# First-weight products by one level of Strassen with seven products, and the batches in two groups, in an attention and two-layer feed-forward kernel on Trainium2

## The chip, the cores and the metric

The kernel runs on one core of one Trainium2 chip. The metric is device time in microseconds (us). Engines are named as in the profile: PE is TensorE (PEld its weight loads), DVE is VectorE, ACT is ScalarE, POOL is GpSimd, and SP (SPq) issues the DMAs.

## The reference

```python
kv = einsum('bhsd,bhse->bhde', k, v)           # batch 4, heads 8, seq 576, head_dim 64
out = einsum('bhsd,bhde->bhse', q, kv)
out = out / sqrt(mean(out * out, -1) + 1e-6) * g_norm
x = out as (2304 tokens, 512)
h = x @ w_in;  x = (h * sigmoid(h)) @ w_out    # layer 1: 512 -> 2048 -> 512
x = ((x @ w_a) * (x @ w_b)) @ w_out2           # layer 2: 512 -> 1536 (twice) -> 512
```

All tensors are float32. On the chip every feed-forward product is made of three matmuls of type fp32r: each operand is split into a rounded high part and a rest, and high*high, high*rest and rest*high are summed.

## The kernel before

**Attention** comes first, for all 18 token tiles of 128 (PE loop at L460): q is transposed (L344), K^T V is made per head pair (L330), multiplied with q (L358), normalised on DVE and ACT, and transposed back (L369) into xT, which holds the 2304 tokens as 6 blocks of 384. K^T V and q times K^T V are plain float32 matmuls; each appears as two instructions in the trace.

**Weights** are loaded by SP (L230) and split by POOL (L309 rounds to the high part, L311 subtracts for the rest), 68 units of 128x512, each once. Both parts stay in SBUF for all blocks.

**Layer 1** runs block by block. For each of 16 slices of 128 hidden columns, the hidden product (L383) is 12 matmuls of 384 columns into one PSUM bank; ACT takes the sigmoid (L546), DVE multiplies (L680), ACT rounds (L551), DVE subtracts (L683), and 12 matmuls (add1, L408) add the slice's share of the output into four PSUM banks that hold the block's sum. The hidden product runs two slices ahead of add1. **Layer 2** is the same with two hidden products per slice (w_a, w_b), 12 slices, and an output product (L434 to L436) of 9 matmuls of 512 columns per slice in which the tokens are the stationary side. Between blocks ACT rounds the next x (L540) and DVE forms its rest (L674). The results are stored by SP.

In all, the hidden products of layer 1 are 1152 matmuls of 384 columns (16 slices x 6 blocks x 12), those of layer 2 1728, add1 1152, and layer 2's output 648 of 512 columns.

## Time and profile before

| | us |
|---|---|
| median of 3 runs (lowest, highest) | 950.91 (947.35, 951.45) |
| span of the profiled execution | 950.9 |
| first matmul of the output product of layer 1 | 97.99 |
| last matmul starts | 947.37 |

The profiled execution's own time is its span, 950.9 us, and it equals the median. The profile gives for each engine the time in which it was busy, and for groups of like instructions the number, the mean duration and what ended the idle time before them. A matmul's row lasts longer than the distance to the next one's start, because matmuls are pipelined; what a matmul costs in a stream is the distance between starts.

### The profile page before, as it was taken

Reading aid. Unit: us, or ns where it says so; the run is one execution under the profiler, and the core shown is the slowest. Engines: PE = TensorE matmul, PEld = TensorE weight load, DVE = VectorE, ACT = ScalarE, POOL = GpSimd, SP = SyncE. Lnnn points to the kernel's source line nnn. Section 1 sums busy time; section 2 is a strip of 40 time slices with the busy share of each in tenths; the row PEclk is TensorE's granted clock in tenths of the full one; section 3 lists DMA queues with packets and bytes.
Section 4 is the critical chain, followed back from the end, with each engine's and each line's share of the span. In section 5 each row is a group of like instructions: output and inputs, shape, how many; then the busy total and the mean of one; then the engine's idle time right before and its main releaser. Section 6 shows DMA issues by size and latency. Waiting matters only on the chain.

```text
span 950.9 us, 13550 instructions
## 1 busy us (share of the span) xinstructions
PE 922.1 (97%) x5368; PEld 885.4 (93%) x5368; DVE 267.4 (28%) x492; ACT 239.6 (25%) x480; POOL 135.9 (14%) x142
## 2 busy tenths in 40 slices
PE   4988899999999999999999999999999999999998
PEld 3977899999999999999989999999999999999997
DVE  1467323223224223233232122112112112112111
ACT  2354323223223223222222122112112112112111
POOL 0039880000000000007990000000000000000000
PEclk8898999999999999999999999999999999999999
DMA  9984440000000000003430000001000000000000
GB/s 218 257 189 125 120 122 1 0 0 0 0 0 0 0 0 0 0 0 88 123 111 1 1 1 33 0 0 33 0 0 33 0 0 33 0 0 8 26 1 34
DMA packets 41881, 37.06 MB, mean 39 GB/s; under 512 B 4224, under 2 KB 36992, under 8 KB 41856
## 3 DMA queue, kind: packets, MB, share of 16 engines
q1 hardware_dynamic: 41856, 36.71, 14.8%
q8 instruction: 18, 0.29, 0.1%
q14 instruction: 7, 0.06, 0.0%
HBM read 31.98 MB, written 4.72 MB: 39 GB/s over the span
## 4 chain that ended last, share of the span: by engine, by line
PE 91%; SPq 3%; DMA 2%; DVE 2%; issue 1%; ACT 1%; ACTq 0%
PE ps L376 25%; PE ps L378 24%; PE ps L377 24%; PE ps L435 5%; PE ps L436 5%; PE ps L434 5%; SPq L245 1%; SPq L237 1%; DMA q_sb<-in_q_dram 1%; DMA v_sb<-in_v_dram 1%; PE ps L358 1%; PE ps L330 1%; DVE x_lo L674 1%; DVE stat L653 0%; PE ps L344 0%
## 5 line engine op out<-in xcount | busy, mean ns | idle before, releaser
L680 DVE TENSOR_TENSOR gate<-gate,ps 128x384 f32<-128x384 f32 x168 | 93.1, 554 | 383.3 <-ACT gate L546 383.3
L546 ACT ACTIVATE gate<-ps 128x384 f32<-128x384 f32 x168 | 82.7, 492 | 394.9 <-PE ps L378 394.9
L376 PE MATMUL ps<-x_hi,w_hi_top 128*128 128x384 f32 x504 | 169.9, 337 | 1.6 <-DVE x_lo L674 1.6
L378 PE MATMUL ps<-x_hi,w_lo_top 128*128 128x384 f32 x504 | 169.4, 336 | 0.0
L377 PE MATMUL ps<-x_lo,w_hi_top 128*128 128x384 f32 x504 | 169.2, 336 | 0.0
L683 DVE TENSOR_TENSOR g_lo<-gate,g_hi 128x384 fp32r<-128x384 f32 x168 | 94.5, 563 | 245.3 <-ACT g_hi L551 245.3
L376 PE MATMUL ps<-x_hi,w_hi_low 128*128 128x384 f32 x456 | 153.8, 337 | 2.3 <-DVE x_lo L674 2.3
L378 PE MATMUL ps<-x_hi,w_lo_low 128*128 128x384 f32 x456 | 153.1, 336 | 0.0
L377 PE MATMUL ps<-x_lo,w_hi_low 128*128 128x384 f32 x456 | 153.0, 336 | 0.0
L551 ACT CAST g_hi<-gate 128x384 fp32r<-128x384 f32 x168 | 86.3, 514 | 252.0 <-PE ps L378 139.0
L376 PEld LDWEIGHTS ps<-x_hi,w_hi_top 128*128 128x128 f32 x504 | 95.1, 189 | 5.0 <-DVE x_lo L674 2.2
L377 PEld LDWEIGHTS ps<-x_lo,w_hi_top 128*128 128x128 f32 x504 | 95.2, 189 | 1.5
L378 PEld LDWEIGHTS ps<-x_hi,w_lo_top 128*128 128x128 f32 x504 | 95.0, 189 | 0.0
L376 PEld LDWEIGHTS ps<-x_hi,w_hi_low 128*128 128x128 f32 x456 | 86.0, 189 | 4.4 <-POOL w_lo_low L311 1.7
L377 PEld LDWEIGHTS ps<-x_lo,w_hi_low 128*128 128x128 f32 x456 | 86.0, 189 | 1.0
L378 PEld LDWEIGHTS ps<-x_hi,w_lo_low 128*128 128x128 f32 x456 | 86.0, 189 | 0.0
L309 POOL TENSOR_SCALAR w_hi_low<-stage 128x512 fp32r<-128x512 f32 x32 | 20.6, 644 | 355.6 <-PE ps L378 293.5
L376 PE MATMUL ps<-g_hi,w_hi_low 128*128 128x384 f32 x192 | 64.8, 338 | 2.4 <-DVE g_lo L683 2.4
L377 PE MATMUL ps<-g_lo,w_hi_low 128*128 128x384 f32 x192 | 64.9, 338 | 0.0
L378 PE MATMUL ps<-g_hi,w_lo_low 128*128 128x384 f32 x192 | 64.8, 337 | 0.0
L378 PE MATMUL ps<-g_hi,w_lo_top 128*128 128x384 f32 x192 | 64.2, 334 | 0.0
L376 PE MATMUL ps<-g_hi,w_hi_top 128*128 128x384 f32 x192 | 64.1, 334 | 0.0
(59 smaller groups left out, 1071.1 us busy)
## 6 DMA issues: line engine op xcount, KB each, us to landing
stage<-in_moe_w_out_dram SPq DMA_DIRECT2D x28, 256.0 KB, 2.6
k_sb<-in_k_dram SPq DMA_DIRECT2D x16, 288.0 KB, 9.1
v_sb<-in_v_dram SPq DMA_DIRECT2D x16, 288.0 KB, 11.0
stage<-in_moe_w_in_dram SPq DMA_DIRECT2D x16, 256.0 KB, 2.7
q_sb<-in_q_dram SPq DMA_DIRECT2D x4, 768.0 KB, 11.5
stage<-in_moe_w_a_dram SPq DMA_DIRECT2D x12, 256.0 KB, 2.8
stage<-in_moe_w_b_dram SPq DMA_DIRECT2D x12, 256.0 KB, 2.9
out_dram<-xT SPq DMA_DIRECT2D x3, 768.0 KB, 3.3
```

Source lines behind the costliest of these rows:

```text
L237: sp.dma_start(dst[0:KVP, B % 2, 2 * h:2 * h + 2, :], src[B, 2 * h:2 * h + 2].rearrange("h (p t) d -> p h (t d)", t=KVT)).then_inc(kv_in[B ...
L309: nc.gpsimd.tensor_scalar(unit_hi(slot), raw, 1.0, 0.0, ALU.mult, ALU.add).then_inc(w_raw_hi, 1)
L376: pe.matmul(dst, hi[:, cols], moving_hi, start=start, stop=False)
L377: pe.matmul(dst, hi[:, cols], moving_lo, start=False, stop=False)
L378: return pe.matmul(dst, lo[:, cols], moving_hi, start=False, stop=stop)
L434: pe.matmul(dst, g_hi[:, f % 2, cols], unit_hi(slot), start=(f == 0), stop=False)
L435: pe.matmul(dst, g_hi[:, f % 2, cols], unit_lo(slot), start=False, stop=False)
L436: mm = pe.matmul(dst, g_lo[:, f % 2, cols], unit_hi(slot), start=False, stop=(f == F2 - 1))
L546: nc.scalar.activation(gate[:, f % 2, :], ps[:, bank, 0:TOK], func).then_inc(s_ready, 1)
L551: nc.scalar.copy(g_hi[:, f % 2, :], gate[:, f % 2, :]).then_inc(gh_ready, 1)
L680: nc.vector.tensor_tensor(gate[:, f % 2, :], gate[:, f % 2, :], ps[:, bank, 0:TOK], ALU.mult).then_inc(g_full, 1)
L683: nc.vector.tensor_tensor(g_lo[:, f % 2, :], gate[:, f % 2, :], g_hi[:, f % 2, :].bitcast(F32), ALU.subtract).then_inc(g_ready, 1)
```

## The change

The feed-forward part is written anew, and the attention with it.

- **Two groups.** Batches 0 and 1 (1152 tokens) go through attention, layer 1 and layer 2, then batches 2 and 3. The attention of the second group stands inside the pairs 1 to 5 of layer 2 of the first group (PE lines L547 to L580). Every weight is loaded and split twice, once for each group.
- **Strassen.** A hidden product covers a pair of hidden slices (256 columns), the 512 inputs in two halves, and a group's tokens in two halves of 576 (its batches). One level of Strassen (Winograd's form) turns the eight block products into seven. Each of the seven steps (`step`, L419) is 12 matmuls of 288 columns. POOL makes the sums of weights (L324, L327, L330, L337) and splits each of the seven operands (L311, L313) into a ring of four; DVE makes the four sums of x and the seven rests once per layer and group (L833, L837), ACT rounds them (L656). ACT keeps partial sums from PSUM (L683, 3 per product) and DVE adds them (L870, 3 per product).
- **Output products** have no PSUM sum over slices any more: after each pair a tile (6 matmuls, of 288 columns at L467 to L469 in layer 1, of 512 at L489 to L491 in layer 2) goes to one of two banks, and DVE adds it to the running sum in SBUF (L919, L929). Layer 1 has 16 tiles per pair, layer 2 nine.
- Layer 1 has 8 pairs per group, layer 2 has 6 pairs with two products each. The matmuls of all hidden products are 1344 of 288 columns in layer 1 and 2016 in layer 2; the output products are 1536 of 288 and 648 of 512.

The core of the diff:

```diff
-            def hidden(bank, slot, x_first):
-                for c in range(KT):
-                    if x_first is not None:
-                        pe.wait_ge(x_ready, x_first + c + 1)
-                    mm = three(ps[:, bank, 0:TOK], weights(slot), slice(c * P, (c + 1) * P),
-                               x_hi[:, c, :], x_lo[:, c, :], c == 0, c == KT - 1)
-                return mm
...
+    SEGS = [(g, layer) for g in range(GROUPS) for layer in (1, 2)]
+    N_PAIRS = [FF1 // (2 * P) if layer == 1 else FF2 // (2 * P) for _, layer in SEGS]
...
+    STEPS = 7
+    RING = 4
+    RAWS = 2
+    G_HALVES = 3
+    BANK_A, BANK_B, BANK_C, BANK_D = 0, 2, 4, 6
+    STEP_BANK = (BANK_A, BANK_A, BANK_A, BANK_B, BANK_A, BANK_C, BANK_C)
+    STEP_BEGINS = (0, 3, 5)
...
+                n = max(n for n in range(len(SEGS)) if RAW0[n] <= r)
+                layer = SEGS[n][1]
+                p, what = divmod(r - RAW0[n], layer + 1)
+                if what == layer:
+                    sp.wait_ge(d_ready, 2 * (PAIR0[n] + p + 1))
+                else:
+                    sp.wait_ge(w_sum, 4 * (PROD0[n] + layer * p + what + 1))
...
+            def load_heads(G, h):
+                buf, fill = staged(G, h)
+                if G and h == 0:
+                    sp.wait_ge(x_ready, 2 * STEPS)
+                before = PAIRS * G + h - (2 if G == 0 else 1)
+                if before >= 0 and (G, h) != (1, 0):
...
+            for r in range(2, RAW0[-1]):
+                load_raw(r)
+                h, rest = divmod(r - RAW0[1], 3)
+                if rest == 2 and 0 <= h < PAIRS:
+                    load_heads(1, h)
+                if r == RAW0[2] + 5:
+                    sp.wait_ge(flushed, DOWN0[2])
+                    for j in range(TOK_TILES):
+                        store_tile(0, j)
...
+            def ready(u, step, src):
+                n = STEPS * u + step
+                if n >= RING:
+                    pool.wait_ge(prod, n - RING + 1)
+                nc.gpsimd.tensor_scalar(w_hi[:, n % RING], src, 1.0, 0.0, ALU.mult, ALU.add).then_inc(w_high, 1)
+                pool.wait_ge(w_high, n + 1)
+                nc.gpsimd.tensor_tensor(w_lo[:, n % RING], src, w_hi[:, n % RING].bitcast(F32),
+                                        ALU.subtract).then_inc(w_ready, 1)
+            def up(u):
+                r = raw_up(u)
+                pool.wait_ge(raw_in[r % RAWS], 16 * (r // RAWS + 1))
+                w = raw[:, r % RAWS, :].rearrange("p (c n) -> p c n", c=KT)
+                b11, b12, b21, b22 = (w[:, 2 * i:2 * i + 2, j * P:(j + 1) * P] for i in range(2) for j in range(2))
+                t0, t1, t2 = (wt[:, j, :].rearrange("p (c n) -> p c n", c=2) for j in range(3))
+                if u:
+                    pool.wait_ge(w_ready, STEPS * u)
+                nc.gpsimd.tensor_tensor(t0, b12, b11, ALU.subtract).then_inc(w_sum, 1)
+                ready(u, 0, b11)
+                pool.wait_ge(w_sum, 4 * u + 1)
+                nc.gpsimd.tensor_tensor(t1, b22, t0, ALU.subtract).then_inc(w_sum, 1)
+                pool.wait_ge(w_sum, 4 * u + 2)
+                ready(u, 1, t1)
+                nc.gpsimd.tensor_tensor(t2, b22, b12, ALU.subtract).then_inc(w_sum, 1)
+                ready(u, 2, t0)
+                ready(u, 3, b21)
+                ready(u, 4, b22)
+                pool.wait_ge(w_sum, 4 * u + 3)
+                ready(u, 5, t2)
+                pool.wait_ge(w_ready, STEPS * u + 3)
+                nc.gpsimd.tensor_tensor(t0, b21, t1, ALU.subtract).then_inc(w_sum, 1)
+                pool.wait_ge(w_sum, 4 * u + 4)
+                ready(u, 6, t0)
...
+                if pp >= 2:
+                    pool.wait_ge(down, down_end(pp - 2))
...
+                at = (STEPS * u + n) % RING
+                pe.wait_ge(w_ready, STEPS * u + n + 1)
+                if u == PROD0[seg]:
+                    pe.wait_ge(x_ready, STEPS * seg + n + 1)
+                if n in STEP_BEGINS and u:
+                    if layer == 2 and u == prods_of(pp)[1]:
+                        if n == 0:
+                            pe.wait_ge(a_kept, a_count(pp))
+                        else:
+                            pe.wait_ge(added, 3 * (u - 1) + (1 if n == 3 else 3))
+                    else:
+                        pe.wait_ge(g_ready, 4 * (pp - 1) + {0: 2, 3: 1, 5: 4}[n])
+                if n in (1, 2):
+                    pe.wait_ge(part_kept, 3 * u + n)
+                if n == 4:
+                    pe.wait_ge(part_kept, 3 * u + 3)
+                if n == 6:
+                    pe.wait_ge(added, 3 * u + 2)
+                bank, begins = STEP_BANK[n], n in STEP_BEGINS
+                for c in range(2):
+                    hi, lo = w_hi[:, at, c, :], w_lo[:, at, c, :]
+                    for w, x, first, last in ((hi, x_hi, c == 0, False), (hi, x_lo, False, False),
+                                              (lo, x_hi, False, c == 1)):
+                        for s in range(2):
+                            mm = pe.matmul(ps[:, bank + s, 0:PART], w, x[:, n, c, s * PART:(s + 1) * PART],
+                                           start=(begins and first), stop=last, skip_group_check=not begins)
+                mm.then_inc(prod, 1)
...
+                t = down0(pp) + n
+                m, d, s = down_order(pp)[n]
+                bank, at = tile_bank(t), (2 * pp + m) % G_HALVES
...
+                wait_turn(bank)
+                part, cols = slice(at * SEQ + s * PART, at * SEQ + (s + 1) * PART), slice(d * P, (d + 1) * P)
...
+                for n in range(STEPS):
+                    step(u, n)
+                    down1(before, 2 * n)
+                    down1(before, 2 * n + 1)
+                down1(before, 14)
+                down1(before, 15)
...
+                step(ua, 0)
+                tile(0)
+                step(ua, 1)
+                tile(1)
+                step(ua, 2)
+                if old is not None:
+                    o_turn(1, old, 0, 6)
+                    o_turn(1, old, 1, 7)
+                step(ua, 3)
+                if new is not None:
+                    kv(1, new)
+                step(ua, 4)
+                tile(2)
+                if old is not None:
+                    o_turn(1, old, 2, other(2))
+                step(ua, 5)
+                tile(3)
+                step(ua, 6)
+                if new is not None:
+                    q_turn(1, new, 0, 6)
+                    q_turn(1, new, 1, 7)
+                step(ub, 0)
+                tile(4)
+                step(ub, 1)
+                tile(5)
+                step(ub, 2)
+                if new is not None:
+                    q_turn(1, new, 2, 6)
+                    q_kv(1, new, 0, 7)
+                step(ub, 3)
+                if new is not None:
+                    q_kv(1, new, 1, 6)
+                step(ub, 4)
+                tile(6)
+                step(ub, 5)
+                tile(7)
+                step(ub, 6)
+                if new is not None:
+                    q_kv(1, new, 2, other(8))
+                tile(8)
...
+                    act.wait_ge(flushed, DOWN0[seg] - 4)
+                x_round(seg, 0, quad(G, 0, 0))
+                act.wait_ge(x_sum, 4 * seg + 2)
+                x_round(seg, 1, ts[1])
+                x_round(seg, 2, ts[0])
...
+                act.wait_ge(prod, STEPS * u + n + 1)
+                if u:
+                    act.wait_ge(added, 3 * (u - 1) + (1, 3, 2)[n])
+                nc.scalar.copy(halves(kept[:, n, :]), both(BANK_A)).then_inc(part_kept, 1)
...
+                x_add(ts[0], quad(G, 1, 0), quad(G, 1, 1), ALU.add)
+            def x_second(seg):
+                G = SEGS[seg][0]
+                ts = [mat(kvq0, j) for j in range(3)]
+                dve.wait_ge(x_sum, 4 * seg + 1)
+                x_add(ts[1], ts[0], quad(G, 0, 0), ALU.subtract)
+                x_rest(seg, 0, quad(G, 0, 0))
+            def x_third(seg):
+                G = SEGS[seg][0]
+                ts = [mat(kvq0, j) for j in range(3)]
+                x_rest(seg, 1, ts[1])
+                x_rest(seg, 2, ts[0])
+                x_add(ts[2], quad(G, 0, 1), ts[1], ALU.subtract)
+                x_rest(seg, 3, quad(G, 0, 1))
+                x_rest(seg, 4, ts[2])
+                x_add(ts[0], quad(G, 0, 0), quad(G, 1, 0), ALU.subtract)
+                x_rest(seg, 5, ts[0])
+                x_rest(seg, 6, quad(G, 1, 1))
...
+                bank, at, n = ((BANK_B, 0, 3), (BANK_C, 2, 5), (BANK_C, 1, 6))[which]
+                dve.wait_ge(prod, STEPS * u + n + 1)
+                dve.wait_ge(part_kept, 3 * u + at + 1)
+                nc.vector.tensor_tensor(dst, halves(kept[:, at, :]), both(bank), ALU.add).then_inc(added, 1)
...
+            def g_rest(pp, tile):
+                m, f = ((0, 0), (0, 1), (1, 1), (1, 0))[tile]
+                dve.wait_ge(g_high, 4 * pp + tile + 1)
...
+                nc.vector.tensor_tensor(halves(g_at_half(g_lo, pp, m, f)), place(tile),
+                                        halves(g_at_half(g_hi, pp, m, f)).bitcast(F32),
+                                        ALU.subtract).then_inc(g_ready, 1)
...
+                def flush(n):
+                    if plain:
+                        flush1(before, n)
+                for n in range(6):
+                    flush(n)
+                add(u, 0, both(BANK_B))
+                flush(6)
+                silu(pp, 0)
+                flush(7)
+                g_rest(pp, 0)
+                silu(pp, 1)
+                flush(8)
+                flush(9)
+                g_rest(pp, 1)
+                add(u, 1, halves(held[:, 2, :]))
+                flush(10)
+                flush(11)
+                silu(pp, 2)
+                g_rest(pp, 2)
+                flush(12)
+                add(u, 2, both(BANK_C))
+                flush(13)
+                flush(14)
+                silu(pp, 3)
+                flush(15)
+                g_rest(pp, 3)
...
+                if layer == 1:
+                    for n in range(8):
+                        flush1(last, n)
+                    dve.wait_ge(flushed, DOWN0[seg + 1] - 8)
+                    x_first(seg + 1)
+                    for n in range(8, 12):
+                        flush1(last, n)
+                    dve.wait_ge(flushed, DOWN0[seg + 1] - 4)
+                    x_second(seg + 1)
+                    for n in range(12, 16):
+                        flush1(last, n)
+                    dve.wait_ge(flushed, DOWN0[seg + 1])
+                    x_third(seg + 1)
...
+                    dve.wait_ge(x_kept, 2 * UNITS)
+                    x_first(nxt)
+                    flush2(last, 0)
+                    x_second(nxt)
+                    flush2(last, 1)
+                    x_rest(nxt, 1, ts[1])
+                    flush2(last, 2)
+                    x_rest(nxt, 2, ts[0])
+                    flush2(last, 3)
+                    x_add(ts[2], quad(H, 0, 1), ts[1], ALU.subtract)
+                    x_rest(nxt, 3, quad(H, 0, 1))
```

What the order of the instructions shows. **TensorE at the start of layer 1, before** (ident and normed belong to the attention; g is a slice of the hidden layer):

```order
L378 MATMUL ps<-x_hi,w_lo_low 128x384
L369 MATMUL ps<-ident,normed 128x128 x8
L480 UNCONDITIONAL_BRANCH
L402 ISA
L405 ISA
L376 MATMUL ps<-g_hi,w_hi_low 128x384
```

**TensorE in the second pair of layer 1, with the change** (the end of a step, then two output tiles):

```order
L448 MATMUL ps<-x_hi,w_hi 128x288 x2
L448 MATMUL ps<-x_lo,w_hi 128x288 x2
L448 MATMUL ps<-x_hi,w_lo 128x288 x2
L467 MATMUL ps<-g_hi,d_hi 128x288
L468 MATMUL ps<-g_lo,d_hi 128x288
L469 MATMUL ps<-g_hi,d_lo 128x288
```

Where a matmul of 384 columns stood for each pair of weight and token block, there are now two of 288 for the same weights, and the tiles of the pair before stand between the steps.

**VectorE at the end of a block, before** (ISA and REGISTER_ALU rows are addresses and waits):

```order
L680 TENSOR_TENSOR gate<-gate,ps 128x384
L683 TENSOR_TENSOR g_lo<-gate,g_hi 128x384
L673 ISA
L674 ISA
L674 TENSOR_TENSOR x_lo<-xT,x_hi 128x384
L673 REGISTER_ALU
```

**VectorE from layer 1 to layer 2 of a group, with the change** (kvq_65 now holds the sums of x):

```order
L919 TENSOR_TENSOR xy<-xy,ps 128x288 x8
L833 TENSOR_TENSOR kvq_65<-xy 128x1152
L919 TENSOR_TENSOR xy<-xy,ps 128x288 x4
L833 TENSOR_TENSOR kvq_65<-kvq_65,xy 128x1152
L837 TENSOR_TENSOR x_lo<-xy,x_hi 128x1152
L919 TENSOR_TENSOR xy<-xy,ps 128x288 x4
L837 TENSOR_TENSOR x_lo<-kvq_65,x_hi 128x1152 x2
L833 TENSOR_TENSOR kvq_65<-xy,kvq_65 128x1152
L837 TENSOR_TENSOR x_lo<-xy,x_hi 128x1152
```

Four operations of 384 elements have become eleven of 1152, and the sixteen adds of output tiles stand between them.

**VectorE in the first pair of layer 1, with the change**:

```order
L837 TENSOR_TENSOR x_lo<-xy,x_hi 128x1152
L870 TENSOR_TENSOR ps<-kept,ps 128x2x288
L879 TENSOR_TENSOR ps<-held,ps 128x2x288
L905 TENSOR_TENSOR g_lo<-ps,g_hi 128x576
L879 TENSOR_TENSOR ps<-held,ps 128x2x288
L905 TENSOR_TENSOR g_lo<-ps,g_hi 128x576
L870 TENSOR_TENSOR held<-kept,ps 128x576
```

The second add at L870, for which the seventh step on TensorE waits, stands behind five operations of the first half.

## Rows read from the trace of the kernel before

**Rows 1.** The page: span, and busy time of each engine

```profile
span 950.9 us, 13550 instructions
PE 922.1 (97%) x5368; PEld 885.4 (93%) x5368; DVE 267.4 (28%) x492; ACT 239.6 (25%) x480; POOL 135.9 (14%) x142
PE ps L376 25%; PE ps L378 24%; PE ps L377 24%; PE ps L435 5%; PE ps L436 5%; PE ps L434 5%; SPq L245 1%; SPq L237 1%; DMA q_sb<-in_q_dram 1%; DMA v_sb<-in_v_dram 1%; PE ps L358 1%; PE ps L330 1%; DVE x_lo L674 1%; DVE stat L653 0%; PE ps L344 0%
L376 PEld LDWEIGHTS ps<-x_hi,w_hi_top 128*128 128x128 f32 x504 | 95.1, 189 | 5.0 <-DVE x_lo L674 2.2
```

**Rows 2.** Windows: stretch, its us, busy (instructions) per engine, granted clock, DMA

```profile
112.00:480.00 368.00, 368.00 (x2124) 367.94 (x2123) 113.47 (x207) 101.62 (x207) 71.31 (x73) 1.00 0.09 26
490.00:494.00 4.00, 2.55 (x12) 1.62 (x10) 4.00 (x4) 1.18 (x3) 3.92 (x4) 1.00 0.49 131
494.00:498.00 4.00, 3.83 (x13) 3.77 (x14) 0.99 (x2) 0.00 (x0) 3.83 (x4) 0.57 0.25 66
```

**Rows 3.** Timeline of PE in layer 2: start us, us, instruction

```profile
897.57 0.39 PE L434 MATMUL ps<-w_hi_low,g_hi 128*128 128x512 f32 x1
...
899.65 0.33 PE L376 MATMUL ps<-x_hi,w_hi_low 128*128 128x384 f32 x1
```

**Rows 4.** The same at the end of the kernel

```profile
941.44 0.39 PE L434 MATMUL ps<-w_hi_top,g_hi 128*128 128x512 f32 x1
...
947.37 0.39 PE L436 MATMUL ps<-w_hi_top,g_lo 128*128 128x512 f32 x1
```

**Rows 5.** Timeline of PE in the attention

```profile
24.09 2.43 PE L330 MATMUL ps<-v_sb,k_sb 96*64 96x64 f32 x24 [4.60 <-DMA v_sb<-in_v_dram]
...
35.35 1.43 PE L330 MATMUL ps<-v_sb,k_sb 96*64 96x64 f32 x24
36.71 1.16 PE L358 MATMUL ps<-kv_sb,qT_sb 128*128 128x128 f32 x8
37.70 0.60 PE L369 MATMUL ps<-ident,normed 128*128 128x128 f32 x4
38.14 0.60 PE L344 MATMUL ps<-ident,q_tile 128*128 128x128 f32 x4
38.67 1.09 PE L358 MATMUL ps<-kv_sb,qT_sb 128*64 128x128 f32 x16
```

**Rows 6.** The page's DMA issues, KB each and us to landing

```profile
k_sb<-in_k_dram SPq DMA_DIRECT2D x16, 288.0 KB, 9.1
```

**Rows 7.** Groups by form, DVE and ACT: busy us, mean ns of one, idle before

```profile
L680 DVE TENSOR_TENSOR gate<-gate,ps 128x384 f32<-128x384 f32 x168 | 93.1, 554 | 383.3 <-ACT gate L546 383.3
L700 DVE COPY xT<-ps 128x512 f32 x5 | 3.4, 683 | 0.0
L546 ACT ACTIVATE gate<-ps 128x384 f32<-128x384 f32 x168 | 82.7, 492 | 394.9 <-PE ps L378 394.9
L573 ACT COPY xT<-ps 128x512 f32 x5 | 2.9, 587 | 0.3
```

**Rows 8.** POOL's two lines: duration ns min/median/max, first and last start

```profile
L309 POOL TENSOR_SCALAR w_hi_top<-stage x36: 612/622/928, 97.6 to 501.4; 128x512 fp32r<-128x512 f32 x36
L311 POOL TENSOR_TENSOR w_lo_top<-stage,w_hi_top x36: 1274/1294/1694, 98.3 to 502.1; 128x512 fp32r<-128x512 f32 x36
```

**Rows 9.** DVE's line L674 (ns min/median/max), then its timeline between the layers

```profile
L674 DVE TENSOR_TENSOR x_lo<-xT,x_hi x48: 544/553/1644, 78.9 to 871.1; 128x384 fp32r<-128x384 f32 x48
490.03 4.96 DVE L674 TENSOR_TENSOR x_lo<-xT,x_hi 128x384 fp32r<-128x384 f32 x4
```

**Rows 10.** Timeline of PE, the first matmul of add1

```profile
97.99 0.49 PE L376 MATMUL ps<-g_hi,w_hi_low 128*128 128x384 f32 x1 [2.39 <-DVE g_lo L683]
```

1153 lines of the change are left out of this document (649 added, 504 removed).

## The prediction

> **What bounds the kernel now.** I read the page first. TensorE is busy 97% of the span, VectorE 28%, ScalarE 25%, GpSimd 14%, and the chain that ended last is made of TensorE's feed-forward lines [rows 1]. The windows say how dense the middle is: 2124 matmuls in 368 us, 0.1733 us from start to start at 384 columns, at a granted clock of 1.00 [rows 2]. The timeline gives the other shape: nine matmuls of 512 columns take 2.08 us, 0.231 each [rows 3], at the very end 26 take 5.93 us, 0.228 each [rows 4]. The feed-forward part is then 4032 x 0.1733 + 648 x 0.231 = 848 us. Ahead of it lie 98.0 us [rows 10], in which the attention and the first 36 matmuls (6 us) run, and 3.5 us follow the start of the last matmul. 98.0 - 6 + 848 + 3.5 = 944; the other 7 us are waits and stretches at half clock, such as the one between the layers. So only two things can help: fewer columns, and a shorter stretch before the stream starts. All times below are made against the profiled execution, 950.9 us, which equals the median of the runs. A measurement of this kernel can tell about 0.5% from no change, 4.75 us.
>
> **Term 1, the stream.** The change leaves 1344 + 2016 + 1536 = 4896 matmuls of 288 columns and the 648 of 512. In columns, 1,880,000 become 1,742,000. What a 288-column matmul costs is nowhere in the trace. At 384 columns the distance is 13.3 ns over 384/2.4 = 160, at 512 it is 18 over 213.3 in the middle and 15 at the end [rows 2 to 4]. Either the surplus is a share (0.1733/384 = 0.451 ns a column, which gives 0.2311 at 512, just what the middle shows), or it is a fixed 13 to 15 ns per matmul. The first gives 130.0 ns at 288, the second 133.3. I take 130.0, because the 512-column row of the same stretch bears it out. Ends: 128 (the end's 0.228/512 a column) and 135 (120 + 15).
> 84 of the 4896 belong to the first pair of the first group and are counted in term 2, so the stream is 4812 x 0.130 + 648 x 0.231 = 625.6 + 149.7 = 775 us.
>
> The Trainium skill ("TensorE: Matmul & The Clock Gate", Back-to-back issue gap) gives a warm gap of N/2.4 + 2.5 ns, which would be 122.5 ns at 288. The trace disagrees: at 384 the page's formula gives 162.5 and the row 173.3. With the page's gap the sum would be 36 us lower; the row at 384 leaves that under 1%, counted in A.
>
> **Term 2, up to the second pair.** The first keys land about 9.1 us after their issue [rows 6], so K^T V starts near 10. It is 72 instructions of 64 columns, 0.10 us each at half clock and 0.057 at full [rows 5]; those of the change alternate between the two column halves, and where that happens in the trace (128*64, 16 instructions in 1.09 us) the same columns take half the time of 128*128 (8 in 1.16). First head pair: 4 us for it, 4 more to the end of q times K^T V, 18 in all. Each of the next three head pairs is one chain through all engines, since one sq buffer and one turn of the banks link them: three squares with their sums 3, three copies of q 1.6, last transpose and its copy 0.9, two more copies and three normalisations on VectorE 3.6, transpose back 0.4, q times K^T V 2.5; 12 us, 36 for three. The last one's normalisation and copies 6. x is complete at 60 us.
> VectorE then has three operations of 1152 elements before the first step and eight after it. One costs 0.554 at 384 and 0.683 at 512 [rows 7], 1.0 ns an element, so 1.3 at 1152: 4 + 10. The first pair's seventh step waits for the second add, which stands behind add, two multiplies and two rests of the first half, with ScalarE's sigmoid and rounding between: 6.5; then the step, 1.6. With 2 for GpSimd (below): 60 + 24 = **84 us**. Bounds 74 (a chain of 10) and 98 (15, all at half clock).
>
> **Term 3, the second group's attention in layer 2.** 288 K^T V instructions x 0.0285 = 8.2, 72 transposes x 0.11 = 7.9, 144 of q times K^T V x 0.068 = 9.8 [rows 5]: **26 us** on TensorE, beside which nothing is saved. Upper bound 34 without the overlap.
>
> **Term 4, the steady pairs.** Layer 1: TensorE 84 + 96 matmuls, 23.4 us. VectorE 11 operations of 576 at 0.75 and 16 adds of 288 at 0.45, 15.5. ScalarE 11 at 0.64 (0.492 at 384, 0.587 at 512 [rows 7]), 7. GpSimd, with 256 elements at half of the row plus start-up, 0.36 and 0.68 [rows 8]: 11 x 0.68 + 7 x 0.36 + gaps 1 = 11 per product, and 4 for the output weights, 15. Layer 2: TensorE 34.3, VectorE 16.7, GpSimd 26, ScalarE 7. Work on the three engines is hidden by sum; the order costs something. Written out from the end of the fourth step, VectorE reaches the flush of tile 12 at 11.1 us, when tile 14 wants its bank, and that of tile 13 at 12.2, when tile 15 wanted it at 11.9: 0.3 to 0.65 a pair, 14 pairs, **7 us**. In layer 2 the same exercise gives no wait in plain pairs; in the four with attention tile 6 waits 1.2 for ScalarE's second copy of o, and the weights behind the heads' six DMAs in SP's queue may come late: **8 us**.
>
> **Term 5, the hand-offs.** From layer 1 to 2 of a group TensorE has 16 tiles and 14 steps, 34 us. VectorE needs 16 flushes, 11 operations on x at 1.3, then the adds, and tiles 10 and 14 wait for banks behind it (3 us), steps 2, 3 and 7 of the first product and step 7 of the second wait 8. Beside that stands GpSimd: four operations of 384 took 4.96 us instead of 2.2 while it worked [rows 9], 0.7 each, and all of the eleven have two SBUF operands; where GpSimd's operations are shorter I take 3. **14 us**, twice. From group 1 to group 2 x is split between the last flushes: 7.5 and 3 less overlap, **10 us**. After 2.5 busy of 4 us, TensorE ran 4 us at 0.57 [rows 2], 1.7 lost; three such, **5 us**.
>
> **Term 6, the end**: as before, **3.5 us**.
>
> Sum: 84 + 775 + 26 + 7 + 8 + 28 + 10 + 5 + 3.5 = **947 us**, 0.4% below. The narrower and fewer products save 63 us (4032 x 0.1733 = 699 against 4896 x 0.130 = 636), and the half attention ahead of the stream 19 (92 against 84 less the first pair's 11). The second group's attention, the hand-offs and the order pay back 84, where before had waits of 7.
>
> **Rivals.**
> *A, cheap hand-offs.* TensorE's queue of tiles may cover more than I count: VectorE's back-to-back rows overlap, its share in the steady state is under 70%, the attention chain may keep the full clock. Term 2 then is 76, terms 4 and 5 half: 947 - 8 - 26 = 913 to 935, say **925**. Against it speak the operations' lengths, which are rows.
> *B, a fixed surplus per matmul* (slower). TensorE pays 13.3 ns for each matmul whatever its columns. 4812 x 3.3 ns = 16 us more: **963**. The place is every matmul of 288; it decides from about 132 ns on. For it: the last rows show 15 ns at 512, hardly more than at 384 [rows 4]. Against: the middle shows 18 [rows 3].
> *C, VectorE's order sets layer 1.* If an add into SBUF with one operand in PSUM, or a write to PSUM, costs a fifth more than my rows, each pair waits 1.5 to 2 us, and hand-offs take 18: 947 + 18 + 10 = **975**.
> *D, GpSimd bounds layer 2.* If 256 elements cost nearly what 512 do (0.62 and 1.29), a pair takes 11 x 2 x 1.29 + 14 x 0.62 + 4 = 41 us against TensorE's 34: 12 pairs x 7, **1030**. It decides from about 1.0 us for the subtract. Against: nothing in rows 8 separates start-up from length, but 0.62 is half of 1.29 for the same elements.
> *E, weight loads bound TensorE.* A load's row is 189 ns against a distance of 173 [rows 1]. If loads set the pace, 4812 x 0.173 gives **1150**. Transposes follow at 0.11 us, each with its own load [rows 5], so a load needs no more than that. The Trainium skill ("Perfetto Trace Analysis", Identifying the Most-Contended Engine) says to judge TensorE by MFU and the busy share of LDWEIGHTS; that share is 93% here, and the change adds a fifth to the number of loads, so the rule speaks for this rival and against the change.
>
> **How the numbers follow.** Forecast (938 to 956) 38%, A 24%, B 20%, C 12%, D 4%, E 2%. Of the forecast's own 38, 17 lie below 946.2, 20 within 0.5% and 1 above; A is faster; of B one is within 0.5%; C, D and E are slower. Faster 41 to 42%, same 21%, slower 37%. The cases of both signs hold the chance, so the likeliest one's own range is 938 to 956; the range for 8 in 10 runs from the middle of A, 920, to past C, 982.
>
> **What would show it.** Distance of 288-column starts: 0.130 (B: 0.133). Second pair of layer 1 starting near 84. A steady pair of layer 1 in 24 us, of layer 2 in 34 to 35, about 43 with attention. Between the layers of a group 48 us from the first of the last pair's 16 tiles to layer 2's second pair, with VectorE busy through most of it. GpSimd's 256-element subtract 0.68. The prediction is wrong if pairs are spaced by an engine other than TensorE, if TensorE stays cold in the attention, or if the hand-offs take under 6 us.

## The result, and the profile after

The changed kernel takes 994.58 us (median of 4, 992.8 to 998.61) against 949.25 for the kernel before in the same series (4 runs, 947.35 to 951.45): a ratio of 1.0489, 95% interval 1.0456 to 1.0523. It is slower by 45 us where 947 was forecast, and the time lies 13 us above the upper end of the range. The profiled execution spans 990.7 us at a mean granted clock of 0.96 (before 0.986); the rows below are of it.

The page answers [rows 1]: TensorE's share falls from 97% to 90%. VectorE is busy twice as long as before (549.2 us, before 267.4), GpSimd four times (554.6, before 135.9) and ScalarE a fifth longer (285.7, before 239.6); none of them comes near the span.

```profile
span 990.7 us, 16939 instructions
PE 889.8 (90%) x6552; PEld 835.2 (84%) x6552; DVE 549.2 (55%) x889; ACT 285.7 (29%) x469; POOL 554.6 (56%) x839
PE   4838999999948999999995799999996799999998
L448 PE MATMUL ps<-x_hi,w_hi 128*128 128x288 f32 x1120 | 248.9, 305 | 61.0 <-ACT kept L683 41.9
```

The row of busy tenths shows where TensorE is not full: at the start, and at three places further on, each of which is the beginning of a layer. The last row names what ended most of the idle time: ScalarE's copy of a partial sum (`kept`, L683). The list of waits has the same, with how often and the longest (us in total, times, longest):

```profile
PE ps L448 <- ACT kept L683: 41.9, 13, 10.3
PE ps L448 <- DVE held L870: 14.0, 6, 5.7
PE ps L467 <- DVE xy L919: 5.4, 4, 2.0
PE ps L489 <- DVE xy L929: 4.1, 4, 1.5
PE ps L448 <- POOL w_lo L313: 0.2, 1, 0.2
```

GpSimd, the rival bound of layer 2, costs TensorE 0.2 us. The windows answer [rows 2] (stretch, its us, busy us and instructions per engine, granted clock, DMA): seven pairs of layer 1 from the second on, then the hand-off from layer 1 to layer 2, then the one between the groups.

```profile
88.40:260.00 171.60, 171.45 (x1257) 168.60 (x1256) 104.38 (x190) 50.64 (x78) 104.94 (x157) 0.99 0.15 44
260.00:305.10 45.10, 28.65 (x177) 27.10 (x178) 25.70 (x33) 11.09 (x13) 9.97 (x16) 0.85 0.17 43
530.00:568.20 38.20, 23.99 (x126) 21.12 (x125) 23.30 (x26) 13.58 (x16) 14.10 (x20) 0.83 0.09 28
```

The stream is dense (171.45 of 171.6 us), the hand-offs are not (28.65 of 45.1 us, and the granted clock falls to 0.85). The time went to the hand-offs. A part of it is the clock: by the distances between starts, matmuls at half clock cost TensorE some 15 us more than at full clock from 60 us on, 9.5 of them in the three hand-offs; in the kernel before it was some 5 us.

The timeline of TensorE at the start of the stream shows one of them. The first step runs at half clock (0.24 us a matmul, from 60.16 on); then:

```profile
62.70 0.68 PE L448 MATMUL ps<-x_hi,w_lo 128*128 128x288 f32 x2
71.31 0.82 PE L448 MATMUL ps<-x_hi,w_hi 128*128 128x288 f32 x2 [7.93 <-ACT kept L683]
...
81.52 0.42 PE L448 MATMUL ps<-x_hi,w_lo 128*128 128x288 f32 x2
85.43 0.82 PE L448 MATMUL ps<-x_hi,w_hi 128*128 128x288 f32 x2 [3.49 <-DVE held L870]
```

The second step waits 7.93 us for a copy of 0.63 us. ScalarE's own timeline says why: the copy is behind seven roundings of x (L656), and these wait for VectorE's sums of x.

```profile
63.89 1.15 ACT L656 CAST x_hi<-kvq 128x1152 fp32r<-128x1152 f32 x1 [1.85 <-DVE kvq L833]
68.42 1.15 ACT L656 CAST x_hi<-kvq 128x1152 fp32r<-128x1152 f32 x1 [3.38 <-DVE kvq L833]
69.48 1.15 ACT L656 CAST x_hi<-xy 128x1152 fp32r<-128x1152 f32 x1
70.53 0.63 ACT L683 COPY kept<-ps 128x576 f32<-128x576 f32 x1
```

The program says the same: `x_rounds(seg)` issues all seven roundings before the first `part` of the layer's first product, so the copy that frees the bank for step two cannot leave before the last rounding. Every layer of both groups begins so; the four waits for that copy are 7.93, 10.33, 6.74 and 9.71 us, 34.7 together.

What a matmul costs stands in the timeline of the steady part, where rows 3 gave it for the kernel before:

```profile
91.49 0.29 PE L468 MATMUL ps<-g_lo,d_hi 128*128 128x288 f32 x1
...
92.81 0.30 PE L469 MATMUL ps<-g_hi,d_lo 128*128 128x288 f32 x1
92.94 0.42 PE L448 MATMUL ps<-x_hi,w_hi 128*128 128x288 f32 x2
```

Eleven distances in 1.45 us are 0.132 each. Inside the steps of steady pairs the distances are not all alike: most are 131 to 132 ns, and every fourth is 140, so that the mean is 0.1333. A whole steady pair (180 matmuls) is 24.0 us of 0.1333 and takes 24.43. What makes every fourth one longer no run here tells. Rows 2 had 0.1733 at 384 without such a pattern.

### The profile page after: what moved, and what is told of

Read it like the earlier page. It is cut to its first block, busy times and chain, and to the rows that moved or that the text cites. A ratio compares the mean times of both kernels' runs of the same rounds, so it can differ in the third digit from the quotient of the medians.

```text
span 990.7 us, 16939 instructions
## 1 busy us (share of the span) xinstructions
PE 889.8 (90%) x6552; PEld 835.2 (84%) x6552; DVE 549.2 (55%) x889; ACT 285.7 (29%) x469; POOL 554.6 (56%) x839
## 4 chain that ended last, share of the span: by engine, by line
PE 82%; DVE 10%; ACT 3%; issue 2%; DMA 1%; SPq 1%; POOL 0%; ACTq 0%; DVEq 0%; POOLq 0%
PE ps L448 44%; PE ps L467 8%; PE ps L468 7%; PE ps L469 7%; PE ps L489 5%; PE ps L491 4%; PE ps L490 4%; DVE x_lo L837 3%; DVE kvq L833 2%; PE ps L405 2%; ACT g_hi L707 1%; ACT kept L683 1%; DMA raw<-in_moe_w_a_dram 1%; PE ps L415 1%; PE ps L380 1%
## 5 line engine op out<-in xcount | busy, mean ns | idle before, releaser
L448 PE MATMUL ps<-x_hi,w_hi 128*128 128x288 f32 x1120 | 248.9, 305 | 61.0 <-ACT kept L683 41.9
L448 PEld LDWEIGHTS ps<-x_hi,w_hi 128*128 128x128 f32 x1120 | 187.6, 193 | 76.5 <-issue 66.2
L448 PE MATMUL ps<-x_lo,w_hi 128*128 128x288 f32 x1120 | 245.3, 301 | 0.0
L448 PE MATMUL ps<-x_hi,w_lo 128*128 128x288 f32 x1120 | 243.9, 300 | 0.0
L448 PEld LDWEIGHTS ps<-x_hi,w_lo 128*128 128x128 f32 x1120 | 185.7, 194 | 0.0
L448 PEld LDWEIGHTS ps<-x_lo,w_hi 128*128 128x128 f32 x1120 | 184.8, 194 | 0.0
L311 POOL TENSOR_SCALAR w_hi<-raw 128x256 fp32r<-128x256 f32 x120 | 51.6, 430 | 200.1 <-PE ps L448 200.0
L467 PE MATMUL ps<-g_hi,d_hi 128*128 128x288 f32 x512 | 155.4, 303 | 9.0 <-DVE xy L919 5.4
L683 ACT COPY kept<-ps 128x576 f32<-128x576 f32 x120 | 77.0, 641 | 278.7 <-PE ps L448 278.6
L311 POOL TENSOR_SCALAR w_hi<-wt 128x256 fp32r<-128x256 f32 x160 | 70.5, 441 | 147.3 <-PE ps L448 143.3
L469 PE MATMUL ps<-g_hi,d_lo 128*128 128x288 f32 x512 | 151.3, 295 | 0.0
L468 PE MATMUL ps<-g_lo,d_hi 128*128 128x288 f32 x512 | 151.2, 295 | 0.0
L919 DVE TENSOR_TENSOR xy<-xy,ps 128x288 f32<-128x288 f32 x224 | 99.9, 452 | 89.3 <-PE ps L469 88.6
L313 POOL TENSOR_TENSOR w_lo<-wt,w_hi 128x256 fp32r<-128x256 f32 x160 | 118.5, 741 | 13.4
L467 PEld LDWEIGHTS ps<-g_hi,d_hi 128*128 128x128 f32 x512 | 96.9, 189 | 16.4 <-issue 12.2
L929 DVE TENSOR_TENSOR xy<-xy,ps 128x512 f32<-128x512 f32 x90 | 61.6, 685 | 87.3 <-PE ps L491 87.3
L313 POOL TENSOR_TENSOR w_lo<-raw,w_hi 128x256 fp32r<-128x256 f32 x120 | 98.1, 818 | 10.0
L469 PEld LDWEIGHTS ps<-g_hi,d_lo 128*128 128x128 f32 x512 | 96.5, 189 | 0.0
L489 PE MATMUL ps<-d_hi,g_hi 128*128 128x512 f32 x216 | 86.0, 398 | 5.5 <-DVE xy L929 4.1
L491 PE MATMUL ps<-d_hi,g_lo 128*128 128x512 f32 x216 | 84.6, 392 | 0.0
```

What stands on the lines that cost most here:

```text
L311: nc.gpsimd.tensor_scalar(w_hi[:, n % RING], src, 1.0, 0.0, ALU.mult, ALU.add).then_inc(w_high, 1)
L313: nc.gpsimd.tensor_tensor(w_lo[:, n % RING], src, w_hi[:, n % RING].bitcast(F32), ALU.subtract).then_inc(w_ready, 1)
L448: mm = pe.matmul(ps[:, bank + s, 0:PART], w, x[:, n, c, s * PART:(s + 1) * PART], start=(begins and first), stop=last, skip_group_check=no ...
L467: pe.matmul(dst, hi, g_hi[:, f, part], start=(f == 0), stop=False)
L468: pe.matmul(dst, hi, g_lo[:, f, part], start=False, stop=False)
L469: mm = pe.matmul(dst, lo, g_hi[:, f, part], start=False, stop=(f == 1))
```

## Experiments

Times are medians; each ratio is to the kernel before, run on the same chip in the same series. Theory 1: the overshoot is mostly ScalarE's order at the four layer starts, and 16 us the price of a matmul. Rivals: VectorE's order or the length of its operations on x, the second group's attention, an eighth that Strassen does not save.

**e1_act_order: ScalarE copies the partial sums between the roundings.**

```diff
                 x_round(seg, 2, ts[0])
+                part(PROD0[seg], 0)
...
                 x_round(seg, 3, quad(G, 0, 1))
+                part(PROD0[seg], 1)
...
                 x_round(seg, 4, ts[2])
+                part(PROD0[seg], 2)
```

(and the three copies are left out where the layer's first pair had them)

> ScalarE's three copies of partial sums of a segment's first product now stand between its roundings of x instead of behind all seven. Theory 1 (ScalarE's program order holds the second step back: waits of 7.9, 10.3, 6.7 and 9.7 us on the line of the copies): these four waits shrink to under 2 us each; about 6.5 us at the start, 8.5 between the layers of each group and 5.5 between the groups come off, 29 us in all: about 965 us. Rival 2 (VectorE's eleven operations on x set the hand-off whatever ScalarE does): the waits move to the rests of x and to VectorE's adds, and less than 10 us come off: about 988. Rival 3 (GpSimd's operations delay VectorE's): no change, 994.

Measured: 968.81 us (967.63 to 971.32), ratio 1.0226 [1.0184, 1.0269]: 26 us less than the change. The waits for the copy are down to 0.82 us, of which the copy itself is 0.64:

```profile
64.65 0.82 PE L448 MATMUL ps<-x_hi,w_hi 128*128 128x288 f32 x2 [0.82 <-ACT kept L686]
...
68.69 0.82 PE L448 MATMUL ps<-x_hi,w_hi 128*128 128x288 f32 x2 [0.82 <-ACT kept L686]
```

and its list of waits has another row on top:

```profile
PE ps L448 <- DVE held L875: 18.0, 6, 6.7
PE ps L448 <- ACT kept L686: 9.0, 12, 0.8
```

The copies cost 9.0 instead of 41.9 us; the second add of the first product (`held`) costs 18.0 instead of 14.0. Of the 32.9 us, 26 reach the end. Theory 1 holds for its larger part. What is left over the matmuls in the hand-offs is 19.8 and 17.5 us from layer 1 to layer 2 and some 15 between the groups, where the forecast had 14, 14 and 10.

**e2_dve_add: VectorE makes the second add of a layer's first pair ahead of the first half's multiplies and rests.**

```diff
                 add(u, 0, both(BANK_B))
+                if not plain:
+                    add(u, 1, halves(held[:, 2, :]))
...
-                add(u, 1, halves(held[:, 2, :]))
+                if plain:
+                    add(u, 1, halves(held[:, 2, :]))
```

> In each segment's first pair VectorE makes the second add, for which the seventh step waits, before the multiplies and rests of the first half; ScalarE's order is as in the change. Theory: the waits for this add in the first pair (3.5 and 5.7 us in layer 1, 1.5 twice in layer 2, 12 in all) go, and 1 to 3 us come back in the tiles that wait for the later rests: about 985 us. Rival (these waits lie beside others that are longer): no change, 994.

Measured: 1000.32 us (1000.2 to 1000.49), ratio 1.0563 [1.0521, 1.0606]; 6 us slower than the change, where 985 or no change was expected. A miss. The wait for the add shrinks from 3.49 to 0.94 us, but the next pair now begins with another:

```profile
84.13 0.51 PE L448 MATMUL ps<-x_hi,w_hi 128*128 128x288 f32 x2 [0.94 <-DVE held L870]
...
88.40 0.51 PE L448 MATMUL ps<-x_hi,w_hi 128*128 128x288 f32 x2 [2.45 <-DVE g_lo L905]
```

The rests of the first half (`g_lo`), which the move delayed, are what the next product's first step waits for. In layer 2 the second pair waits 2.24 and 2.53 us for a copy of ScalarE, where it waited 0.59 and 0.84, and gets 1.7 and 3.2 us longer. In this order the chain from the first add to the last rest has no room; what is moved ahead in it delays what stands behind.

**e3_both: the two together.**

```diff
+                part(PROD0[seg], 0)
...
+                if not plain:
+                    add(u, 1, halves(held[:, 2, :]))
```

> Both edits. If the two waits lie one behind the other, their gains add: 994 - 29 - 10 = 955 us. If the second is only another name of the first, the time is that of the first edit alone, about 965. If VectorE's sum of work sets the hand-off, it stays above 980.

Measured: 974.17 us (973.83 to 979.52), ratio 1.0304 [1.0252, 1.0355], 5 us slower than e1_act_order alone and neither of the two values expected (955, 965). In layer 1 the first two pairs together gain 1.9 us in one group and 1.8 in the other; in layer 2 the second pairs lose 3.2 each (45.2 and 39.0 instead of 42.0 and 35.8). It bears e2_dve_add out.

**e5_no_attn2: the second group's attention and its loads left out.**

```diff
-                new = p - 1 if G == 0 and 1 <= p <= PAIRS else None
-                old = p - 2 if G == 0 and 2 <= p <= PAIRS + 1 else None
+                new = None
+                old = None
...
+            nc.vector.memset(xy[:, 1, :], 0.5).then_inc(cleared, 1)
```

> Leaves out the attention of batches 2 and 3 and its loads; their x is a constant. Theory (the second group's attention costs TensorE its own time and little more): pairs 2 to 5 of layer 2 of the first group fall from 41.3 to 42.3 us to 34.7, and the time by 4 x 7.1 + 1, to about 965 us. Rival (it also delays weights or VectorE at the hand-off between the groups): more than 35 us come off, below 959. Rival (it fills gaps and costs little): under 15 us come off.

Measured: 967.3 us (966.89 to 967.72), ratio 1.0215 [1.0161, 1.0268]; 27 us less than the change. Layer 2's pairs with attention take 34.7 to 35.5 us instead of 41.3 to 42.1. The change's own timeline has what a head pair's matmuls take by themselves, here for K^T V, for three transposes, and for a third of q times K^T V:

```profile
331.38 1.28 PE L380 MATMUL ps<-kvq 64*64 64x64 f32 x72
348.38 0.49 PE L393 MATMUL ps<-ident,kvq 128*128 128x128 f32 x3
348.80 0.88 PE L405 MATMUL ps<-kv_sb,qT_sb 128*64 128x128 f32 x12
```

From start to start K^T V takes 1.21 us, the nine transposes of q 0.99, q times K^T V 2.42 and the nine transposes of o 0.82: 5.4 us a head pair, 22 for the four. The other 5 us of the 27 are on top. They are waits (0 to 1.5 us a pair, some of them for ScalarE's copies of o) and larger distances of the matmuls beside the attention (23.1 to 23.4 us for a pair's steps instead of 22.3). In sum the attention costs less than the 26 and 8 us forecast; it is not where the forecast failed.

**e6_flush13: e1_act_order, and in the steady pairs of layer 1 VectorE takes tile 13 from its bank ahead of the third add.**

```diff
                 flush(12)
-                add(u, 2, both(BANK_C))
                 flush(13)
+                add(u, 2, both(BANK_C))
```

> The first edit (ScalarE's copies between the roundings), and in the steady pairs of layer 1 VectorE's flush of tile 13 ahead of the third add. Theory (the 0.43 us by which a steady pair of layer 1 exceeds its 180 matmuls is tile 15 waiting for that flush): 14 pairs fall from 24.43 to 24.0 us, 6 us in all, 963 us. Rival (the 0.43 is made of TensorE's own turns of banks or semaphores): still 24.4, 969.

Measured: 965.88 us (964.81 to 967.36), ratio 1.0198 [1.0173, 1.0222]. It is 3 us less than e1_act_order, where 6 were expected. A steady pair takes 24.14 to 24.20 instead of 24.43 us: the wait that the prediction counted for tile 15's bank (0.3 to 0.65 us a pair) is real, and the order undoes somewhat more than half of it.

**e8_short_rests: e1_act_order, with only 16 of 1152 elements of each rest of x for layer 2.**

```diff
+                if seg in (1, 3):
+                    nc.vector.tensor_tensor(x_lo[:, n, :, 0:8], src[:, :, 0:8], x_hi[:, n, :, 0:8].bitcast(F32),
+                                            ALU.subtract).then_inc(x_ready, 1)
+                    return
```

> The first edit, and VectorE's rests of x for layer 2 (seven of 1152 elements for each group) only 16 elements long; the others keep layer 1's values, so the precision of layer 2 is not that of the reference. Theory (after ScalarE's order is mended, VectorE's work on x holds steps 5 to 7 back): the waits for x and the add behind it (2.6, 1.0 us) go and the clock stays up; each hand-off from layer 1 to 2, 79 us for two pairs, falls to about 71: 969 - 16 = 953 us. Rival (what is left are the copies of partial sums between steps without tiles): less than 6 us come off.

Measured: 957.06 us (956.55 to 957.57), ratio 1.0105 [1.0077, 1.0134]; 12 us less than e1_act_order, where 16 were expected. The two pairs across each hand-off to layer 2 take 70.9 us instead of 79.0 and 76.7, where their matmuls need 59.2. So with ScalarE's order mended, 6 to 8 us of each such hand-off hang on the length of VectorE's seven subtracts, and some 12 are there without them. Matmuls at half clock are a part of the 6 to 8: they cost 4.1 and 1.5 us in these places in e1_act_order's trace, and none run at half clock there in this one.

**e7_early_x: e6_flush13 with work on x moved forward.** The first group's x is rounded and summed in part during its attention, the second group's three sums and two rests are made inside the last pair of layer 2, and the first pairs are ordered add, rest, both multiplies, second add, rests of g. It is a rewrite of some 80 lines; the core:

```diff
+                if last:
+                    dve.wait_ge(x_kept, 2 * UNITS)
+                    x_first(2)
+                    dve.wait_ge(x_sum, 9)
+                    x_add(ts[1], ts[0], quad(1, 0, 0), ALU.subtract)
+                    dve.wait_ge(x_sum, 10)
+                    x_add(ts[2], quad(1, 0, 1), ts[1], ALU.subtract)
...
+                if h == 3:
+                    dve.wait_ge(x_kept, 2 * JS)
+                    x_add(held[:, 0:2, :], quad(0, 0, 0), quad(0, 1, 0), ALU.subtract)
```

> Both edits of the run before, and work on x moved to where VectorE is idle: for the first group one sum and one rounding and rest during the attention; for the second group three sums and two rests during the last pair of layer 2 of the first; in the first pair of layer 1 of each group the adds, multiplies and rests stand between and behind the rests of x, with the second add early and ScalarE's two sigmoids first; tile 8 between the last two steps. Theory (the hand-offs are long because single-engine orders put late what TensorE wants next, not because VectorE's sum of work is too large): the first pair ends near 75 us instead of 87, the hand-off between the groups falls by 12 us, and the time is 963 - 12 - 12 = 939 us, below that of the kernel before. Rival (VectorE with GpSimd beside it is simply too slow there): it stays above 955.

Measured: 951.87 us (7 runs, 949.91 to 956.23), ratio 1.0054 [1.0026, 1.0082]; 14 us less than e6_flush13, 13 short of what was expected and also below the rival's 955. The hand-off between the groups, last pair and first pair, goes from 74.1 to 60.9 us (from 79.9 in the change). The run changes many things at once and does not tell what each of them is worth. The start of the stream gains little:

```profile
63.24 0.82 PE L453 MATMUL ps<-x_hi,w_hi 128*128 128x288 f32 x2 [2.32 <-DVE x_lo L885]
...
77.66 0.50 PE L453 MATMUL ps<-x_hi,w_hi 128*128 128x288 f32 x2 [1.35 <-DVE held L918]
...
85.08 0.49 PE L453 MATMUL ps<-x_hi,w_hi 128*128 128x288 f32 x2 [2.40 <-ACT kept L712]
```

The first pair is 4 us shorter than e6_flush13's, the second 3.4 longer, 28.3 us: its copy (L712) stands behind the last rounding of g in ScalarE's queue. The same mistake one pair on.

**e10_attn_order: e7_early_x with another order in the first group's attention.**

```diff
                 if h + 1 < PAIRS:
                     kv(0, h + 1)
+                if h:
+                    for j in range(JS):
+                        o_turn(0, h - 1, j, j)
...
-                if i:
-                    act.wait_ge(ssq, i)
-                nc.scalar.activation(sq[:], ps[:, bank, 0:TILE3], ACT.Square).then_inc(sq_ready, 1)
+                if i > 2:
+                    act.wait_ge(ssq, i if G else i - 2)
+                nc.scalar.activation(sq_buf(G, j), ps[:, bank, 0:TILE3], ACT.Square).then_inc(sq_ready, 1)
```

> The kernel of e7_early_x with another order in the first group's attention: TensorE transposes a head pair's normalised o back (L420) after the next head pair's q times K^T V instead of before it, ScalarE makes the three squares one after the other into three buffers and copies o after them, and takes the transposed-back tiles of the pair before. Theory: a head pair there is a chain through four engines, about 10 us long, of which 2.5 to 3 us is q times K^T V standing behind the normalisation of the pair before; then three periods get 2 to 3 us shorter each, the first step of the stream starts 6 to 8 us earlier, near 50 us instead of 57.7, and the run takes about 945 us. Rival: the chain is set by the sum of VectorE's work (about 6.3 us a head pair) and waits around it, or by the loads of q, k and v; then nothing or under 3 us comes of it, 949 to 952 us. Against the kernel before neither can be told from no change with certainty: 945 would be 0.2 per cent faster.

Measured: 951.98 us (12 runs, 950.47 to 954.97), ratio 1.0042 [1.0025, 1.0059]: nothing gained, the rival's case. One reason is on the timeline:

```profile
22.04 2.19 PE L413 MATMUL ps<-kv_sb,qT_sb 128*64 128x128 f32 x36
27.36 0.89 PE L388 MATMUL ps<-kvq 64*64 64x64 f32 x40 [3.14 <-DMA kvq<-in_v_dram]
```

TensorE is ready for the third head pair's K^T V some 3 us before v is there; later the copies wait for one another on ScalarE. Which of loads and copies would decide with the other gone was not tried.

**e4_step_twice: the change with each product's fourth step done twice,** as an eighth block product would be.

```diff
-                for c in range(2):
+                for c in (0, 1, 0, 1) if n == 3 else (0, 1):
```

> The change with the fourth step of every product done twice (the second time from a cleared bank, so that the result is the same): eight steps where Strassen has seven. Theory (a step in the stream costs its 12 matmuls, 12 x 0.1333 = 1.6 us, 40 products): 994 + 64 = 1058 us, less what falls into waits of the four first pairs, up to 8: 1050 to 1058. Rival (the three idle engines' work bounds the pairs): under 1030.

Measured: 1060.22 us (1059.61 to 1060.84), ratio 1.1194 [1.1163, 1.1226]; 66 us more than the change. 480 matmuls of 0.1333 us are 64.0, and a steady pair of layer 1 takes 26.03 instead of 24.43 us, 12 matmuls of 0.1333 more. So 0.1333 us is what a matmul of 288 columns costs in this stream. The seventh-for-eighth of Strassen is worth in full what it should be in this kernel; what it saves is spent elsewhere.

**e9_narrow and e11_cols256: e1_act_order with fewer columns in the eight matmuls of a step that hold a rest.**

```diff
+                        cols = PART if w is hi and x is x_hi else 192
                         for s in range(2):
-                            mm = pe.matmul(ps[:, bank + s, 0:PART], w, x[:, n, c, s * PART:(s + 1) * PART],
+                            mm = pe.matmul(ps[:, bank + s, 0:cols], w, x[:, n, c, s * PART:s * PART + cols],
```

> The kernel of e1_act_order in which the eight matmuls of a step that hold a rest (high times rest, rest times high) read and write only 192 of the 288 columns of each half; the other 96 get the product of the high parts alone, so a part of the small terms is left out. 2240 matmuls change. Two theories of a matmul's price. Fixed surplus of 13.3 ns per matmul (rival B of the prediction): the distance from a start to the next is 192/2.4 + 13.3 = 93.3 ns at 192 columns, a step takes 4 x 0.1333 + 8 x 0.0933 = 1.28 us instead of 1.60, a steady pair of layer 1 takes 2.2 us less (about 22.2), and the run is 2240 x 0.040 = 90 us shorter where TensorE sets the pace, about 880 to 890 us if the hand-offs keep their length. A surplus that is a share of the columns (0.451 ns a column from the 384-column row of before, 0.463 from the 288-column row of the change): 87 to 89 ns, steps of 1.23 us, 95 to 105 us shorter. If weight loads set a floor (PEld rows of some 190 ns), distances do not fall under 133 ns at all and the time stays near 969 us.

Measured: 936.04 us (935.73 to 936.35), ratio 0.9867 [0.9832, 0.9902], 33 us less than e1_act_order where 80 to 105 were expected. Both theories miss. The timeline, two matmuls to a row:

```profile
112.23 0.42 PE L449 MATMUL ps<-x_hi,w_hi 128*128 128x288 f32 x2
112.49 0.36 PE L449 MATMUL ps<-x_lo,w_hi 128*128 128x192 f32 x2
112.69 0.39 PE L449 MATMUL ps<-x_hi,w_lo 128*128 128x192 f32 x2
112.91 0.45 PE L449 MATMUL ps<-x_hi,w_hi 128*128 128x288 f32 x2
```

The rows of 192 columns take 0.20 and 0.22 us for two. But the row of 288 columns behind them takes 0.29 instead of 0.26, so the two rows by themselves flatter the price. Over a pair, 56 narrowed matmuls save 1.1 us in layer 1 (23.3 instead of 24.43) and 112 save 2.34 in layer 2 (32.36 instead of 34.70), which leaves 0.112 to 0.113 a matmul, not 0.093. Something else than columns holds them at about the 0.11 us of the transposes [rows 5]. It is not a floor of 0.133, the third case of the expectation. The same edit with 256 in the place of 192 lies above it:

> As e9_narrow, with 256 instead of 192 of 288 columns in the eight matmuls of a step that hold a rest; the other 32 columns of each half get the product of the high parts alone. In e9_narrow the distances at 192 columns came out at 110 to 113 ns, where a fixed surplus gives 93.3 and a share 87 to 89: something of about 111 ns holds each matmul, as in the transposes, which also follow at 0.11 us. 256 columns lie above that by either theory. Fixed surplus: 256/2.4 + 13.3 = 120.0 ns; a share: 0.451 to 0.463 ns a column, 115.5 to 118.5 ns; with the floor added to rather than compared with the columns (a rounding off between the two) 122 to 125 ns. A steady pair of layer 1 has 56 such matmuls: 24.43 - 56 x 0.0133 = 23.7 us by the fixed one, 23.4 to 23.6 by a share; the run about 968.8 - 2240 x 0.0133 = 939 to 950 us.

Measured: 943.73 us (7 runs, 942.15 to 946.27), ratio 0.993 [0.9909, 0.9951], 25 us less than e1_act_order; a steady pair takes 23.65 us.

```profile
112.62 0.42 PE L449 MATMUL ps<-x_hi,w_hi 128*128 128x288 f32 x2
112.88 0.40 PE L449 MATMUL ps<-x_lo,w_hi 128*128 128x256 f32 x2
113.12 0.40 PE L449 MATMUL ps<-x_hi,w_lo 128*128 128x256 f32 x2
113.35 0.43 PE L449 MATMUL ps<-x_hi,w_hi 128*128 128x288 f32 x2
```

Over layer 1's steady stretch the 256-column starts are 118.4 ns apart and the 288-column starts of the same steps 131.8: 13.4 ns for 32 columns, 0.42 a column. The expectation had 120.0 ns for a fixed surplus and 115.5 to 118.5 for a share of the columns, and for the pair 23.7 us and 23.4 to 23.6. The 118.4 ns lie at the upper end of the share's range, the 23.65 us between the two, so the run does not decide. What the distance has over columns/2.4 is 11.7 ns at 256 columns, 11.8 at 288 in this run, 13.3 at 384 and 15 to 18 at 512: neither the same everywhere nor a constant share. In this run the longer fourth distance is missing; in the change it is 140 ns and makes the mean 133.3. The 33 us at 192 columns and 25 at 256 also say that below 256 little more is to be had: 64 columns fewer give 8 us for 2240 matmuls.

No version that computes all that the reference asks for beats the kernel before; the nearest are e7_early_x and e10_attn_order, 0.5% and 0.4% above it. e9_narrow and e11_cols256 are shorter than the kernel before only because they leave small terms out.

## Why the prediction was wrong

The forecast's terms against the trace of the change:

| term | forecast | measured | difference |
|---|---|---|---|
| 1, stream, per 288-column matmul | 0.130 | 0.1333, 4812 times | +16 |
| 2, start of the second pair | 84 | 88.4 | +4 |
| 3 and 4, attention inside layer 2 | 26 + 8 | 27 (e5_no_attn2), of it 22 its own matmuls | -7 |
| 4, steady pair of layer 1, over its matmuls | 0.3 to 0.65 | 0.43 | -1 |
| 5, two hand-offs from layer 1 to 2 | 28 | 25.8 + 24.6 | +22 |
| 5, between the groups | 10 | about 20 | +10 |
| 5, clock of the hand-offs (9.5 us, inside the two rows above) | 5 | 0 | -5 |
| 6, end | 3.5 | 4.5 | +1 |

A hand-off's figure is the length of the layer's first and the last layer's last pair less their matmuls (85.0 us less 59.2; 83.8 less 59.2; 79.9 less about 59). The sum is 40 of the 43.7 us between 947 and the span; the second pairs of layer 1 (25.7 and 25.2 us instead of 24.4) hold 2 more.

**The step that failed is term 5, the hand-offs.** It counted VectorE's work ("16 flushes, 11 operations on x at 1.3, then the adds") and took a copy of ScalarE's as made whenever it was wanted. For steps 2, 3 and 7 of the first product and step 7 of the second together it had a wait of 8 us; step 2 alone waited 10.3 and 9.7. ScalarE was busy 29% of the time, but its queue is in the order of the program, and the copy that step two of every layer's first product waits for came eighth, behind roundings that themselves waited for VectorE. Four waits of 7 to 10 us came of it, and e1_act_order, which changes only that order, takes 26 us off. With it the three hand-offs still cost some 14 us more than forecast. The length of VectorE's work and the half clock that comes with the waits are in that rest (e8_short_rests); how it divides further stays open. The same order is in term 2; there a shorter attention (x complete near 56 us, not 60) hid most of it.

**Term 1 was mis-sized by 16 us.** The prediction had 133.3 ns as rival B, at 963 us, with 20%, and chose 130.0, a share of the columns, since 0.451 ns a column from the 384-column rows also gave 0.2311 at 512. Measured is a mean of 133.3, and e4_step_twice adds steps at that price. So B's price is right and worth the 16 us it named; its mechanism, the same surplus for each matmul, is not shown. Three of four distances are 131 to 132 ns, between the two readings, and the fourth is 140, which neither had; that the mean equals B's figure is in part luck. By itself the price did not decide the case. With e1_act_order's 26 us gone the change would stand at 969, 6 above B's 963.

**What held, and what fell.** The second group's attention cost 27 us where terms 3 and 4 had 34. Its own matmuls were taken too dear, 26 us for 22, mostly K^T V (2.05 us a head pair for 1.21), and some 5 us came on top where term 4 had 8. Steady pairs are set by TensorE: 24.43 us in layer 1, 34.7 in layer 2, 41.3 to 42.1 with attention, where 24, 34 to 35 and 43 were forecast. Rival A fell with the hand-offs. Rival C fell: steady pairs wait 0.4 us, not 1.5 to 2. Rival D fell: GpSimd's operations of 256 elements take 0.41 and 0.74 us at the median, 65% and 57% of those of 512 in [rows 8], and 0.2 us of TensorE's waits come of them. Rival E, the weight loads, fell: a load's row is still 193 ns long while matmuls start every 133. The Trainium skill ("Perfetto Trace Analysis", Identifying the Most-Contended Engine) judges TensorE by MFU and the busy share of LDWEIGHTS. The trace agrees in so far as that share fell from 93% to 84% as the time went up; the share of before did not warn of this, since the loss came from waits that no share of before contained.

**Why the saving is gone.** Forecast was a saving of 63 us from narrower and fewer products. At 0.1333 a matmul, 699 us become 653, a saving of 46, and the stretch ahead of the stream is 15 shorter (92 against 88.4 less 11.2 of matmuls); 7 us of waits of before go too. Against these 68 stand 27 us of attention, 70 of the three hand-offs, 6 of steady waits and 2 of second pairs, 105 in all: 37 of the 39.8 us by which the profiled span grew. The two groups double the number of layer starts, and each of the three hand-offs costs 20 us or more, since all tokens of a group cross a layer at once; the kernel before crosses block by block.

## What to carry to other kernels

At a place where a stage begins, write down for every engine, the little used ones too, what stands in its queue before the one short operation that the next stage waits for, and put that operation as early as its inputs allow, unless it pushes back work on a chain without room (e2_dve_add). Where a change adds stage starts, price one by such a list and not by sums of busy time. A matmul's price at a width that no row shows is uncertain: here a line through the two known widths, 384 and 512, gives 130 ns at 288, the mean was 133.3, and at 192 the price stopped falling near 0.11 us. With thousands of matmuls, carry both ends of that uncertainty into the sum, or time one run at the new width.
